# A decayed-attention kernel whose keys and queries come from the host also by dimension, with the decay powers made by doubling

## Chip, cores and metric

The kernel runs on one core of a Trainium2 chip. The metric is the device time of one launch in microseconds, before against after. It does attention and then two mixture-of-experts layers, in one program.

## What is computed

Only the attention part is touched by the change. B = 2 batches, H = 8 heads, S = 768 tokens, D = 48 dimensions, all float32:

```python
state = zeros(B, H, D, D)
for t in range(S):
    cur = einsum('bhd,bhe->bhde', u * k[t], v[t])
    y[t] = einsum('bhd,bhde->bhe', r[t], state + cur)
    state = w[..., None] * state + einsum('bhd,bhe->bhde', k[t], v[t])
```

Its result, as rows of B * S tokens by 384, goes through a layer of 8 experts with one expert to a token, and then through a second one with a capacity.

## The kernel before

The program is written engine by engine, with semaphores set by hand. Each engine's instructions run in the order in which its block writes them.

**Units.** Attention is cut into 12 units of 128 tokens (`NU` = 12); unit n is batch n % 2, chunk n // 2. `units` (L355) writes units 0 to 3 out and loops over the rest, four to a pass. A ring of four buffers holds the loaded r, k and v, 192 KB each, by token (`k_raw`, `r_raw`, `v_raw`; `load`, L403). The heads stand in four pairs g, and in a pair j = 0, 1 lie in partitions 0 to 47 and 64 to 111.

**What a unit does.** With decay w per dimension, a chunk is computed as matrices: k times w to a negative power and r times w to a positive one, so that their product holds the decay between two tokens.

- POOL (GpSimd), L553: `prod1` = r u, `prod2` = `prod1` k, then `r_sc` = r times a table of powers for the next unit (`scale_r`, L546), then `sc`, the diagonal matrices of the bonus of all eight heads, 128x1024 (L568).
- DVE (VectorE), L842: `bonus` = sum of `prod2` over dimensions (L813), `k_sc` for the next unit (L807), `st_sum` (L819) = state plus the update in PSUM, the causal mask, which copies the scores over the lower part of `sc` (L832), and the state's decay (L825).
- PE (TensorE), L1122: turns of `k_sc` and `r_sc` into PSUM (`turn_kr`, L1068 and L1072), the rows of unit n - 2 (L1090), the state update (L1081), the state's part of the values (L1100), the masked scores' part (L1106), the scores of unit n (L1118).
- ACT (ScalarE), L708: copies the turned k and r from PSUM (`kT`, `rT`), the finished rows (`x_rows`, `lg_parts`) and `yT`; in units 1 to 3 it also rounds a third of the first expert's second weight (`w_hi`, `split_high`), for which it waits on the load of that weight.

**Who waits for whom.** `bonus` of unit n waits for `prod2` of n and for the diagonal of n - 1, which read the same tile; the diagonal of n waits for `bonus` of n. The mask of n waits for the scores and the diagonal of n; the values of n for the mask. POOL's `prod1` of n + 1 waits for `bonus` of n.

**Setup.** POOL clears and fills constants; DVE makes the powers with four scans and a reciprocal (L787, L790); PE turns them and ACT copies them to two tables (`k_tab`, `r_tab`). 50 bf16 matmuls ahead of it (`keep_clock`) have no other use than to keep PE busy. Behind attention the routing of layer 1 starts from the last rows.

## Time and profile before

| what | us |
|---|---|
| median of 3 runs | 395.46 (395.17 to 395.58) |
| the profiled execution, whole | 396.4 |
| its span | 394.3 |
| of it PE busy | 366.7 (93%) |
| POOL busy | 184.5 (47%) |
| DVE busy | 209.6 (53%) |
| ACT busy | 133.0 (34%) |

The span is from the first to the last instruction that the profiler saw; the execution's own time is 2.1 us more. An engine's busy share is a mean over stages of different kinds: attention (some 0 to 82 us of the span), the routing, and the two layers. An instruction that waits inside the engine, after its semaphores, counts as busy in its row.

### The profile page before, as it was taken

The page shows a single profiled execution, that of the slowest core. Times are in us where ns is not written, and L with a number is a line of the kernel's source. Part 1 is how long each engine was busy: PE and PEld are TensorE (multiplying, and loading weights), DVE is VectorE, ACT ScalarE, POOL GpSimd, SP SyncE. Part 2 cuts the span into 40 slices and gives each one's busy share as a digit, 9 for nine tenths or more (in the row PEclk, how much of TensorE's full clock was granted, in tenths as well). Part 3 has the DMA queues.
Part 4 walks back from the last instruction along what each step waited for, and adds up shares of the span by engine and source line. Part 5 has one row for each costly group of instructions (what it writes and reads, how often), then busy time and mean ns, then how long its engine had stood idle before and what let it go on. Part 6 is the DMA issues. An engine that isn't in the chain of part 4 may idle for free.

```text
span 394.3 us, 10784 instructions
## 1 busy us (share of the span) xinstructions
PE 366.7 (93%) x3406; PEld 356.9 (91%) x3407; DVE 209.6 (53%) x539; ACT 133.0 (34%) x230; POOL 184.5 (47%) x303
## 2 busy tenths in 40 slices
PE   4689999988999999999999999879999999999990
PEld 4579999977899999999999999769999999999990
DVE  4356666689688655555555577474214454244210
ACT  2447554410544222222222252105215555255220
POOL 6798999815455532323232334152434524444311
PEclk9999999998999999999999999699999999999996
DMA  6898774146999511111111321139349998492000
GB/s 128 142 353 185 164 161 100 40 129 169 402 405 404 215 40 40 40 40 40 40 40 40 112 114 40 13 82 403 122 153 350 317 327 299 136 345 98 27 23 17
DMA packets 68238, 62.08 MB, mean 157 GB/s; under 512 B 45493, under 2 KB 61028, under 8 KB 68080
## 3 DMA queue, kind: packets, MB, share of 16 engines
q1 hardware_dynamic: 63904, 51.26, 40.9%
q0 software_dynamic: 3744, 10.23, 7.9%
q8 instruction: 17, 0.28, 0.3%
q10 hardware_dynamic: 560, 0.21, 0.2%
q14 instruction: 13, 0.11, 0.1%
HBM read 52.85 MB, written 10.14 MB: 160 GB/s over the span
## 4 chain that ended last, share of the span: by engine, by line
PE 82%; DMA 6%; SPq 4%; DVE 3%; issue 2%; ACT 1%; POOL 1%; ACTq 0%; POOLq 0%; DVEq 0%
PE p_h L1203 35%; PE p_o L1225 28%; DMA w_sb<-in_moe_w 3%; PE p_sc L1118 3%; SPq L406 3%; PE p_x L1090 3%; PE p_xt L1180 2%; PE p_y L1100 2%; PE p_y L1106 2%; DMA w_raw<-in_moe_w 2%; PE p_kv L1081 1%; PE p_kt L1068 1%; PE p_rt L1072 1%; PE p_o L1050 1%; DMA xg<-x_rows,src_idx 1%
## 5 line engine op out<-in xcount | busy, mean ns | idle before, releaser
L1203 PE MATMUL p_h<-xT,w_sb 128*128 128x128 f32 x1296 | 149.3, 275 | 1.6 <-ACT xT L670 1.0
L1203 PEld LDWEIGHTS p_h<-xT,w_sb 128*128 128x128 f32 x1296 | 148.2, 192 | 2.3 <-issue 1.3
L982 DVE SCALAR_TENSOR_TENSOR h_lo<-p_h,h_hi 128x512 fp32r<-128x512 f32 x54 | 37.4, 692 | 78.9 <-ACT h_hi L753 77.8
L999 DVE CUSTOM_DVE_ANT_0 lg_prod<-y_row,wg_all 128x384 f32<-128x384 f32 x112 | 55.8, 554 | 41.9 <-ACT y_row L763 41.7
L1225 PE MATMUL p_o<-w_hi,h_hi 128*128 x216 | 75.4, 349 | 0.0
L1225 PE MATMUL p_o<-w_lo,h_hi 128*128 x216 | 73.1, 339 | 0.0
L1225 PE MATMUL p_o<-w_hi,h_lo 128*128 x216 | 73.0, 338 | 0.0
L753 ACT ACTIVATE h_hi<-p_h 128x512 fp32r<-128x512 f32 x54 | 32.3, 598 | 112.2 <-PE p_h L1203 112.2
L580 POOL TENSOR_TENSOR dst_mark<-zeros 128x1 f32<-128x1 f32 x54 | 15.7, 290 | 105.8 <-DVE y_row L999 68.6
L839 DVE TENSOR_TENSOR w_lo<-w_raw,w_hi 128x1024 fp32r<-128x1024 f32 x36 | 42.0, 1221 | 7.8 <-ACT w_hi L670 7.8
L580 POOL TENSOR_TENSOR src_mark<-zeros 128x1 f32<-128x1 f32 x54 | 18.8, 348 | 49.1 <-PE p_xt L1180 33.9
L1225 PEld LDWEIGHTS p_o<-w_hi,h_hi 128*128 128x128 f32 x216 | 40.6, 188 | 0.3 <-issue 0.2
L1225 PEld LDWEIGHTS p_o<-w_lo,h_hi 128*128 128x128 f32 x216 | 40.6, 188 | 0.0
L1225 PEld LDWEIGHTS p_o<-w_hi,h_lo 128*128 128x128 f32 x216 | 40.5, 188 | 0.0
L763 ACT ACTIVATE y_row<-p_o,gate_slot 128x384 f32<-128x384 f32 x27 | 15.7, 582 | 69.0 <-PE p_o L1225 69.0
L670 ACT ACTIVATE w_hi<-w_raw 128x1024 fp32r<-128x1024 f32 x36 | 35.8, 1056 | 4.1 <-DMA w_raw<-in_moe_w 3.8
L595 POOL DMA_INDIRECT xg<-x_rows,src_now x27 | 29.8, 1102 | 6.1 <-issue 4.5
L568 POOL TENSOR_TENSOR sc<-ident,bonus 128x1024 f32<-128x1024 f32 x12 | 25.9, 2162 | 0.8 <-DVE bonus L813 0.8
L832 DVE COPY_PREDICATED sc<-causal,p_sc 128x1024 f32<-128x1024 int32 x12 | 16.0, 1335 | 11.4 <-POOL sc L568 11.4
L670 ACT ACTIVATE xT<-p_xt 128x384 f32<-128x384 f32 x29 | 14.1, 487 | 18.8 <-PE p_xt L1180 18.5
L1050 PE MATMUL p_o<-before_b,ones_b 128*128 128x128 bf16 x254 | 19.2, 244 | 0.9 <-DVE last_tile L949 0.9
L607 POOL DMA_INDIRECT x_rows<-y_row,dst_now x15 | 15.2, 1013 | 8.5 <-issue 8.5
(183 smaller groups left out, 408.9 us busy)
## 6 DMA issues: line engine op xcount, KB each, us to landing
...
k_raw<-in_k SPq DMA_DIRECT2D x12, 192.0 KB, 3.2
r_raw<-in_r SPq DMA_DIRECT2D x12, 192.0 KB, 3.6
v_raw<-in_v SPq DMA_DIRECT2D x12, 192.0 KB, 3.8
x_rows<-x_rows SPq DMA_DIRECT2D x12, 192.0 KB, 1.9
...
```

The source lines that it names most:

```text
L568: gp.tensor_tensor(sc[b][:, :, :, :], ident[:, :].unsqueeze(1).unsqueeze(2).broadcast_to([P, 2, HP, T]), bonus[:, :].rearrange("p (g j) -> ...
L580: gp.tensor_tensor(of[:, :], zeros[:, 0:1], zeros[:, 0:1], ALU.add).then_inc(signal, 1)
L595: gp.indirect_dma_start(out=xg[par][:, 0:width], out_offset=None, in_=src[:, :], in_offset=bass.IndirectOffsetOnAxis(ap=rows, axis=0))\
L670: copy = lambda o, i: sa.activation(o, i, ACT.Copy)
L753: sa.activation(h_hi[:, n * FH:(n + 1) * FH, :], p_h[n][:, :, :], ACT.Relu).then_inc(h_high[layer], 1)
L832: nv.copy_predicated(sc[b][:, :, :, :], low, p_sc[:, :, :, :]).then_inc(masked, 1)
L839: tt(w2_lo[:, at:at + PCW], w2_raw[place][:, n * PCW:(n + 1) * PCW], w2_hi[:, at:at + PCW].bitcast(F32), ALU.subtract).then_inc(w2_ready, 1)
L982: stt(h_lo[:, at, :], p_h[n][:, :, :], 0.0, h_hi[:, at, :].bitcast(F32), ALU.max, ALU.subtract).then_inc(h_ready[layer], 1)
L999: last = nv.tensor_tensor_reduce(out=lg_prod[:, n, :], in0=y_row[par][:, 0:DM], in1=wg2_all[:, e, :], op0=ALU.mult, op1=ALU.add, scale=1.0 ...
L1050: mm(at[:, 0:P], ones_b[:, :], before_b[:, :], start=(n == 0), stop=(n == count - 1))
L1203: last = mm(p_h[half][:, f, :], w1_sb[place][:, c, col:col + P], xT[:, c, :], start=(c == 0), stop=(c == DC - 1))
L1225: last = mm(p_o[:, 0:DM], lhs[:, f, :], rhs[:, here], start=(f == 0 and m == 0), stop=(f == FC - 1 and m == 2))
```

## The change

- The host lays r, k and v side by side by token (`rkv`, one DMA of 128 x 4608 bytes a unit into `nat`), and k and r a second time by dimension (`kr_by_dim`, into `krT`, 112 partitions x 4096 bytes). w comes already one to a partition, in one DMA.
- PE no longer turns k and r. DVE makes `kT` and both halves of `rT` from `krT` and tables of powers, all in SBUF. The state update needs k by token still: `k_sc` moves from DVE to POOL; `r_sc` goes.
- The diagonal is halved: POOL makes j = 0, ACT j = 1 with four activations whose scale is a column of `bonus`. The decay moves from DVE to ACT, four activations a unit, and `st_sum` becomes `acc`, one to a batch.
- `mask` of unit n comes in DVE's unit n + 1, ahead of `kT` and `rT` of n + 1. PE starts a unit with rows(n - 2).
- The powers are made by six doublings (`grow`). ACT copies them into `pr` and `pk`; only `pk` is turned, behind the first scores.
- Clearing is dealt out between DVE and POOL; `zeros`, `ones_e` and the iotas are made by POOL behind attention. `w_hi` of the first expert is made by ACT behind attention.

Where the instructions stand now. DVE, one unit of the loop over units, before (rows between the instructions are register and wait work):

```order
L813 TENSOR_REDUCE bonus<-prod 128x8
L807 TENSOR_TENSOR k_sc<-k_raw,k_tab 128x8x48
L819 TENSOR_TENSOR st_sum<-st,p_kv 128x192
L829 REGISTER_ALU
L831 MEMSET gate_in 128x1
L832 COPY_PREDICATED sc<-causal,p_sc 128x1024
L823 REGISTER_ALU
L825 TENSOR_TENSOR st<-st_sum,pw 128x4x48
```

and now:

```order
L822 TENSOR_REDUCE bonus<-prod 128x8
L835 MEMSET gate_in 128x1
L836 COPY_PREDICATED sc<-causal,p_sc 128x1024
L807 TENSOR_TENSOR kT<-krT,pk 112x512
L814 TENSOR_TENSOR rT<-krT,pr 48x512 x2
L828 TENSOR_TENSOR acc<-st,p_kv 128x192
```

`k_sc` and the decay are gone, and `kT` and two `rT` stand between the mask and the state's sum. POOL, one unit of the loop, before:

```order
L555 TENSOR_TENSOR prod<-r_raw,u_tab 128x384
L556 ISA
L557 TENSOR_TENSOR prod<-prod,k_raw 128x384
L548 ISA
L550 TENSOR_TENSOR r_sc<-r_raw,r_tab 128x8x48
L566 REGISTER_ALU
L53 REGISTER_ALU
L568 TENSOR_TENSOR sc<-ident,bonus 128x1024
```

and now:

```order
L537 TENSOR_TENSOR prod<-nat,u_tab 128x384
L538 ISA
L539 TENSOR_TENSOR prod<-prod,nat 128x384
L543 REGISTER_ALU
L53 REGISTER_ALU
L545 TENSOR_TENSOR sc<-ident,bonus 128x512
L552 TENSOR_TENSOR k_sc<-nat,k_tab 128x8x48
```

`r_sc` is gone, `k_sc` stands last, and the diagonal has 512 columns in place of 1024. PE, from its first matmuls to the scores of the first unit before:

```order
L1050 MATMUL p_x<-before_b,ones_b 128x128 x50
L1057 MATMUL p_kt<-ident,pk 128x112 x4
L1057 MATMUL p_rt<-ident,pr 128x112 x4
L1068 MATMUL p_kt<-ident,k_sc 112x128 x4
L1072 MATMUL p_rt<-ident,r_sc 112x128 x4
L1050 MATMUL p_x<-before_b,ones_b 128x128 x12
L1118 MATMUL p_sc<-rT,kT 128x128 x8
```

and now to the scores of the second:

```order
L1071 MATMUL p_warm<-before_b,ones_b 128x128 x50
L1131 MATMUL p_sc<-rT,kT 128x128 x8
L1081 MATMUL p_tab<-ident,pk 128x112 x4
L1071 MATMUL p_warm<-before_b,ones_b 128x128 x12
L1109 MATMUL p_y<-rT,st 64x128 x8
L1119 MATMUL p_y<-sc,nat 64x128 x8
L1091 MATMUL p_kv<-nat,k_sc 64x48 x8
L1131 MATMUL p_sc<-rT,kT 128x128 x8
```

The scores of unit 0 (the first L1131) now stand ahead of the only turn of powers (L1081).

The diff, cut to its core:

```diff
-                for to, src in ((k_raw[q][:, :, :], k_t), (r_raw[q][:, :, :], r_t), (heads(v_raw[q]), v_t)):
-                    sp.dma_start(to, src[b, bass.ds(c, 1), :, :, :].rearrange("n t h d -> (n t) h d"))\
-                        .then_inc(raw_loaded[q], 16)
+                sp.dma_start(nat[q][:, 0:3 * W], rkv_t[b, bass.ds(c, 1), :, :].rearrange("n t x -> (n t) x"))\
+                    .then_inc(nat_loaded[q], 16)
+                sp.dma_start(krT[q][0:R, :, :, :], kr_t[b, bass.ds(c, 1), :, :, :, :].rearrange("n p x g t -> (n p) x g t"))\
+                    .then_inc(krT_loaded[q], 16)
...
-                    sp.wait_ge(r_scaled, n + 1)
+                    sp.wait_ge(kT_ready, n + 1)
+                    sp.wait_ge(rT_ready, n + 1)
...
+            def products(i, q, n):
+                pool.wait_ge(nat_loaded[q], 16 * (i + 1))
+                wait_pos(pool, bonus_sum, n)
+                gp.tensor_tensor(prod1[:, :, :], r_nat(q), u_tab[:, :, :], ALU.mult).then_inc(bonus_prod, 1)
+                pool.wait_ge(bonus_prod, 2 * n + 1)
+                gp.tensor_tensor(prod2[:, :, :], prod1[:, :, :], k_nat(q), ALU.mult).then_inc(bonus_prod, 1)
+            def diagonal(n, b):
+                pool.wait_ge(bonus_sum, n + 1)
+                wait_pos(pool, y_made, n - 1)
+                gp.tensor_tensor(sc[b][:, 0, :, :], ident[:, :].unsqueeze(1).broadcast_to([P, HP, T]),
+                                 bonus[:, :].rearrange("p (g j) -> p j g", j=2)[:, 0, :].unsqueeze(2).broadcast_to([P, HP, T]),
+                                 ALU.mult).then_inc(diag_pool, 1)
+            def scale_k(q, n, b):
+                wait_pos(pool, kv_made, n - 1)
+                gp.tensor_tensor(k_sc[b][:, :, :, 0:D], k_nat(q).rearrange("p (g j) d -> p g j d", j=2),
+                                 k_tab[:, :, :, 0:D], ALU.mult).then_inc(k_scaled, 1)
+            def unit(i, q, n, b, c):
+                products(i, q, n)
+                if isinstance(n, int) and n == 0:
+                    pool.wait_ge(cleared, 2)
+                    pool.wait_ge(k_tab_ready, 1)
+                    scale_k(q, n, b)
+                else:
+                    diagonal(n, b)
+                    scale_k(q, n, b)
+            pool.wait_ge(u_loaded, 16)
+            units(pool, unit)
...
-                wait_pos(pool, bonus_sum, n)
-                gp.tensor_tensor(prod1[:, :, :], r_raw[q][:, :, :], u_tab[:, :, :], ALU.mult).then_inc(bonus_prod, 1)
-                pool.wait_ge(bonus_prod, 2 * n + 1)
-                gp.tensor_tensor(prod2[:, :, :], prod1[:, :, :], k_raw[q][:, :, :], ALU.mult).then_inc(bonus_prod, 1)
-                if q < RING - 1:
...
-                pool.wait_ge(bonus_sum, n + 1)
-                wait_pos(pool, y_made, n - 1)
-                gp.tensor_tensor(sc[b][:, :, :, :], ident[:, :].unsqueeze(1).unsqueeze(2).broadcast_to([P, 2, HP, T]),
-                                 bonus[:, :].rearrange("p (g j) -> p j g", j=2).unsqueeze(3).broadcast_to([P, 2, HP, T]),
-                                 ALU.mult).then_inc(bonus_diag, 1)
...
+            act.dma_start(u_tab[:, :, :], u.partition_broadcast(P)).then_inc(u_loaded, 16)
...
+            act.wait_ge(grown, 7)
+            copy(pr[:, :, M + 1:T], grow[:, 0, :, 0:M - 1])
+            copy(pr[:, :, 0:M], grow[:, 1, :, M - 1::-1]).then_inc(powers_ready, 1)
+            copy(pk[:, :, M:T], grow[:, 1, :, :])
+            copy(pk[:, :, 0:M - 1], grow[:, 0, :, M - 2::-1]).then_inc(powers_ready, 1)
+            act.wait_ge(powers_turned, 1)
+            copy(k_tab[:, :, :, :].rearrange("p g j d -> p g (j d)")[:, :, 0:R], p_tab[:, :, 0:R]).then_inc(k_tab_ready, 1)
...
+            def decay(n, b):
+                act.wait_ge(summed, n + 1)
+                act.wait_ge(y_made, n + 1)
+                for g in range(HP):
+                    last = sa.activation(st[b][:, g, 0:D], acc[b][:, g, :], ACT.Copy, scale=w_T[:, g:g + 1])
+                last.then_inc(decayed, 1)
+            def diagonal(n, b):
+                act.wait_ge(bonus_sum, n + 1)
+                wait_pos(act, y_made, n - 1)
+                for g in range(HP):
+                    last = sa.activation(sc[b][:, 1, g, :], ident[:, :], ACT.Copy, scale=bonus[:, 2 * g + 1:2 * g + 2])
+                last.then_inc(diag_act, 1)
...
-                copy(kT[0:R, :, :], p_kt[0:R, :, :]).then_inc(kT_ready, 1)
-                wait_pos(act, y_made, n - 1)
-                for j in range(2):
-                    at = slice(HD * j, HD * j + D)
-                    last = copy(rT[b][at, j, :, :], p_rt[at, :, :])
...
+                diagonal(n, b)
                 if not (isinstance(n, int) and n < 2):
                     rows(n - 2, b, c - 1)
                 if not (isinstance(n, int) and n < 1):
                     y_out(n - 1)
-                if isinstance(n, int) and 0 < n <= NPC:
-                    split_high(0, 0, [n - 1])
+                    decay(n - 1, 1 - b)
...
+            split_high(0, 0)
...
-            def scale_k(i, q, n, b):
-                dve.wait_ge(raw_loaded[q], 48 * (i + 1))
-                wait_pos(dve, kv_made, n - 1)
-                tt(k_sc[b][:, :, :, 0:D], pairs(k_raw[q]), k_tab[:, :, :, 0:D], ALU.mult).then_inc(k_scaled, 1)
...
+            dve.wait_ge(w_loaded, 16)
+            nv.tensor_copy(grow[:, 0, :, 0:1], w_col[:, :].unsqueeze(2))
+            nv.reciprocal(grow[:, 1, :, 0:1], w_col[:, :].unsqueeze(2)).then_inc(grown, 1)
+            for n in range(6):
+                m = 1 << n
+                dve.wait_ge(grown, n + 1)
+                tt(grow[:, :, :, m:2 * m], grow[:, :, :, 0:m], grow[:, :, :, m - 1:m].broadcast_to([P, 2, HP, m]),
+                   ALU.mult).then_inc(grown, 1)
+            dve.wait_ge(grown, 7)
+            dve.wait_ge(cleared, 2)
+            def scale_kT(i, q, n, b):
+                dve.wait_ge(krT_loaded[q], 16 * (i + 1))
+                wait_pos(dve, scored, n - 1)
+                tt(kT[b][0:R, :, :], krT[q][0:R, 0, :, :], pk[0:R, :, :], ALU.mult).then_inc(kT_ready, 1)
+            def scale_rT(q, n, b):
+                wait_pos(dve, y_made, n - 1)
+                for j in range(2):
+                    at = slice(HD * j, HD * j + D)
+                    last = tt(rT[b][at, j, :, :], krT[q][at, 1, :, :], pr[at, :, :], ALU.mult)
+                last.then_inc(rT_ready, 1)
...
-                wait_pos(dve, bonus_diag, n)
+                wait_pos(dve, diag_pool, n)
+                wait_pos(dve, diag_act, n)
...
-            def state_decay(n, b):
-                dve.wait_ge(state_ready, 2 * n + 1)
-                dve.wait_ge(y_made, n + 1)
-                tt(st[b][:, :, 0:D], st_sum[:, :, :], decay, ALU.mult).then_inc(state_ready, 1)
+                wait_pos(dve, decayed, n - 1)
+                tt(acc[b][:, :, :], st[b][:, :, 0:D], p_kv, ALU.add).then_inc(summed, 1)
...
+                dve.wait_ge(diag_act, n + 1)
...
             def unit(i, q, n, b, c):
-                bonus_of(n)
-                if q < RING - 1:
-                    scale_k(i, q + 1, n + 1, 1 - b)
+                if isinstance(n, int) and n == 0:
+                    dve.wait_ge(krT_loaded[0], 16)
+                    tt(kT[0][0:R, :, M:T], krT[0][0:R, 0, :, M:T], grow[0:R, 1, :, :], ALU.mult)
+                    tt(kT[0][0:R, :, 0:M - 1], krT[0][0:R, 0, :, 0:M - 1], grow[0:R, 0, :, M - 2::-1], ALU.mult)
+                    nv.tensor_copy(kT[0][0:R, :, M - 1:M], krT[0][0:R, 0, :, M - 1:M]).then_inc(kT_ready, 1)
+                    dve.wait_ge(powers_ready, 1)
+                    scale_rT(q, n, b)
+                    bonus_of(n)
+                    tt(w_T[:, :], grow[:, 0, :, M - 1], grow[:, 0, :, M - 1], ALU.mult)
+                    dve.wait_ge(bonus_sum, 1)
+                    dve.wait_ge(consts, 2)
+                    tt(sc[0][:, 0, :, :], ident[:, :].unsqueeze(1).broadcast_to([P, HP, T]),
+                       bonus[:, :].rearrange("p (g j) -> p j g", j=2)[:, 0, :].unsqueeze(2).broadcast_to([P, HP, T]),
+                       ALU.mult).then_inc(diag_pool, 1)
+                elif isinstance(n, int) and n == 1:
+                    dve.wait_ge(powers_ready, 2)
+                    scale_kT(i, q, n, b)
+                    mask(n - 1, 1 - b)
+                    scale_rT(q, n, b)
+                    state_sum(n - 1, 1 - b)
+                    bonus_of(n)
                 else:
-                    if isinstance(i, int):
-                        scale_k(i + 1, 0, n + 1, 1 - b)
-                    else:
-                        with dve.If(i < NU // RING - 1):
-                            scale_k(i + 1, 0, n + 1, 1 - b)
-                if not (isinstance(n, int) and n < 1):
+                    bonus_of(n)
+                    mask(n - 1, 1 - b)
+                    scale_kT(i, q, n, b)
+                    scale_rT(q, n, b)
                     state_sum(n - 1, 1 - b)
-                mask(n, b)
-                if not (isinstance(n, int) and n < 1):
-                    state_decay(n - 1, 1 - b)
-            scale_k(0, 0, 0, 0)
             units(dve, unit)
-
+            mask(NU - 1, (NU - 1) % B)
+            dve.wait_ge(consts, 3)
...
-                    last = turn(p_t[:, g, 0:R], t[0:R, g, :], ident[0:R, 0:R])
+                    last = turn(p_tab[:, g, 0:R], pk[0:R, g, :], ident[0:R, 0:R])
...
-                pe.wait_ge(raw_loaded[q], 48 * (i + 1))
+                wait_pos(pe, summed, n)
+                pe.wait_ge(nat_loaded[q], 16 * (i + 1))
...
-            def values(q, n, b):
-                pe.wait_ge(rT_ready, n + 1)
-                wait_pos(pe, state_ready, 2 * n - 2)
+            def inter(n, b):
+                wait_pos(pe, decayed, n - 1)
...
+            def values(i, q, n, b):
+                pe.wait_ge(nat_loaded[q], 16 * (i + 1))
                 pe.wait_ge(masked, n + 1)
...
-                        last = mm(p_sc[:, j, g, :], kT[at, g, :], rT[b][at, j, g, :], start=True, stop=True)
+                        last = mm(p_sc[:, j, g, :], kT[b][at, g, :], rT[b][at, j, g, :], start=True, stop=True)
...
-                turn_kr(n, b)
                 if isinstance(n, int) and n == 0:
-                    keep_clock(p_x[:, 0, :], WARM_TURN)
-                if not (isinstance(n, int) and n < 2):
+                    score(n, b)
+                    turn_powers()
+                    keep_clock(p_warm[:, 0, :], WARM_TURN)
+                elif isinstance(n, int) and n == 1:
+                    inter(n - 1, 1 - b)
+                    values(0, 0, n - 1, 1 - b)
+                    state(0, 0, n - 1, 1 - b)
+                    score(n, b)
+                else:
+                    before = i if q else i - 1
+                    if isinstance(n, int) and n == 2:
+                        pe.wait_ge(small_in, 16 * N_SMALL)
+                        pe.wait_ge(cleared, 2)
                     rows(n - 2)
-                if not (isinstance(n, int) and n < 1):
-                    state(i if q else i - 1, (q - 1) % RING, n - 1, 1 - b)
-                    values((q - 1) % RING, n - 1, 1 - b)
-                score(n, b)
+                    state(before, (q - 1) % RING, n - 1, 1 - b)
+                    inter(n - 1, 1 - b)
+                    values(before, (q - 1) % RING, n - 1, 1 - b)
+                    score(n, b)
...
+    laid = {"rkv": np.stack([r, k, v]).transpose(1, 3, 0, 2, 4)}
+    rows = np.arange(HD) % D
+    kr = np.stack([k, r]).reshape(2, B, H // 2, 2, S // T, T, D).transpose(1, 4, 3, 6, 0, 2, 5)
+    laid["kr_by_dim"] = kr[:, :, :, rows].reshape(B, S // T, 2 * HD, 2, H // 2, T)[:, :, 0:HD + D]
+    laid["w_by_dim"] = w.reshape(H // 2, 2, D).transpose(1, 2, 0)[:, rows].reshape(2 * HD, H // 2)
```

## Rows read from the trace of the kernel before

**Rows 1.** Busy time by stretch: start:end us, length, PE, PEld, DVE, ACT, POOL, PEclk, DMA.

```profile
10.00:20.00 10.00, 6.85 (x88) 5.71 (x90) 3.58 (x7) 4.31 (x8) 8.01 (x7) 1.00 0.82 141
...
50.00:60.00 10.00, 10.00 (x156) 9.33 (x152) 6.74 (x12) 5.22 (x12) 9.84 (x9) 1.00 0.68 144
```

**Rows 2.** Chain that ended last: start us, length us, engine, tile and line.

```profile
16.86 8.38 DMA w_raw<-in_moe_w
...
26.22 0.59 ACT kT L670
...
27.98 1.16 PE p_sc L1118 x16
...
60.21 1.09 PE p_sc L1118 x16
61.30 0.58 PE p_kt L1068 x4
61.88 0.44 PE p_rt L1072 x4
62.32 0.89 PE p_x L1090 x8
...
65.57 1.09 PE p_sc L1118 x16
...
76.29 1.09 PE p_sc L1118 x16
```

**Rows 3.** Timeline, POOL and DVE in one unit: start, length, engine, line, operation.

```profile
60.00 2.22 POOL L568 TENSOR_TENSOR sc<-ident,bonus 128x1024 f32<-128x1024 f32 x1
...
62.17 1.00 POOL L555 TENSOR_TENSOR prod<-r_raw,u_tab 128x384 f32<-128x384 f32 x1
...
63.25 1.01 POOL L557 TENSOR_TENSOR prod<-prod,k_raw 128x384 f32<-128x384 f32 x1
63.56 0.91 DVE L825 TENSOR_TENSOR st<-st_sum,pw 128x192 f32<-128x192 f32 x1
...
64.22 1.12 POOL L550 TENSOR_TENSOR r_sc<-r_raw,r_tab 128x384 f32<-128x384 f32 x1
...
64.86 0.89 DVE L807 TENSOR_TENSOR k_sc<-k_raw,k_tab 128x384 f32<-128x384 f32 x1
65.30 2.21 POOL L568 TENSOR_TENSOR sc<-ident,bonus 128x1024 f32<-128x1024 f32 x1
```

**Rows 4.** Timeline, the same instructions where the other engine is quiet.

```profile
11.62 0.56 DVE L807 TENSOR_TENSOR k_sc<-k_raw,k_tab 128x384 f32<-128x384 f32 x1 [1.30 <-ACT r_tab L670]
...
15.03 0.99 POOL L550 TENSOR_TENSOR r_sc<-r_raw,r_tab 128x384 f32<-128x384 f32 x1
...
15.10 0.55 DVE L813 TENSOR_REDUCE bonus<-prod 128x8 f32<-128x384 f32 x1 [2.92 <-POOL prod L557]
...
75.61 1.90 POOL L568 TENSOR_TENSOR sc<-ident,bonus 128x1024 f32<-128x1024 f32 x1 [0.76 <-DVE bonus L813]
...
78.86 0.33 DVE L825 TENSOR_TENSOR st<-st_sum,pw 128x192 f32<-128x192 f32 x1
```

**Rows 5.** Instructions by line on DVE: operation, shapes, count, busy us, mean ns.

```profile
L839 DVE TENSOR_TENSOR w_lo<-w_raw,w_hi 128x1024 fp32r<-128x1024 f32 x36 | 42.0, 1221 | 7.8 <-ACT w_hi L670 7.8
...
L832 DVE COPY_PREDICATED sc<-causal,p_sc 128x1024 f32<-128x1024 int32 x12 | 16.0, 1335 | 11.4 <-POOL sc L568 11.4
...
L819 DVE TENSOR_TENSOR st_sum<-st,p_kv 128x192 f32<-128x192 f32 x11 | 3.8, 342 | 0.0
...
L780 DVE MEMSET k_sc<- 128x512 f32 x2 | 1.0, 485 | 1.0 <-PEq L1272 0.9
```

**Rows 6.** Issues of DMAs: KB each, us to landing.

```profile
k_raw<-in_k SPq DMA_DIRECT2D x12, 192.0 KB, 3.2
```

**Rows 7.** Timeline, end of attention and ScalarE's next wait.

```profile
82.64 0.19 ACT L670 ACTIVATE lg_parts<-p_x 128x32 f32<-128x32 f32 x1
...
86.07 0.21 ACT L670 ACTIVATE plan_ends<-ends 1x8 int32<-1x8 f32 x1 [3.25 <-DVE ends L905]
```

More of the change, by code:

```diff
@@ L164, in chain_program @@
             gate_in = sa("gate_in", [P, 1])
-            st_sum = sa("st_sum", [P, HP, D])
+            acc = [sa(f"acc{b}", [P, HP, D]) for b in range(B)]
             st = [sa(f"st{b}", [P, HP, HD]) for b in range(B)]
@@ L280, in chain_program @@
         cleared = sem("cleared")
-        raw_loaded = [sem(f"raw_loaded{q}") for q in range(RING)]
-        r_scaled = sem("r_scaled")
+        krT_loaded = [sem(f"krT_loaded{q}") for q in range(RING)]
+        nat_loaded = [sem(f"nat_loaded{q}") for q in range(RING)]
         k_scaled = sem("k_scaled")
@@ L348, in chain_program @@
         wg2_spread = sem("wg2_spread")
[L350 to L351 removed]
+        N_SMALL, N_ROUTER = 2, 4
+        W = H * D
+        part = lambda q, x: nat[q][:, x * W:(x + 1) * W].rearrange("p (h d) -> p h d", d=D)
+        r_nat, k_nat, v_nat = (lambda q: part(q, 0)), (lambda q: part(q, 1)), (lambda q: part(q, 2))
         rows_of = lambda j: slice(HD * j, HD * j + HD)
[L353 removed]
         def units(eng, unit):
@@ L572, in _ @@
-            pool.wait_ge(tables_ready, 2)
-            scale_r(0, 0, 0, 0)
-            units(pool, unit)
+            pool.wait_ge(consts, 3)
+            pool.wait_ge(zeros_set, 1)
             def mark(of, signal):
@@ L778, in _ @@
             over_c = lambda a, n: a.unsqueeze(1).broadcast_to([P, n, a.shape[1]])
-            for t in k_sc:
-                last = nv.memset(t[:, :, :, :], 0.0)
-            last.then_inc(cleared, 1)
-            dve.wait_ge(consts, 1)
-            dve.wait_ge(w_loaded, 32)
-            nv.memset(pw[:, :, 0:1], 1.0)
-            for g in range(HP):
-                last = nv.tensor_tensor_scan(pw[:, g, 1:T + 1], w_col[:, g:g + 1].broadcast_to([P, T]),
-                                             zeros[:, 0:T], 1.0, ALU.mult, ALU.add)
@@ new lines, in _ @@
+            nv.memset(eye_wg1[:, :, :], 0.0).then_inc(ones_set, 1)
+            nv.memset(k_sc[0][:, :, :, :], 0.0)
+            for t in st:
+                nv.memset(t[:, :, :], 0.0)
+            for q in range(RING):
+                nv.memset(nat[q][:, 3 * W:], 0.0)
+            nv.memset(pr[:, :, M:M + 1], 1.0)
+            nv.memset(pk[:, :, M - 1:M], 1.0).then_inc(cleared, 1)
+            dve.wait_ge(w_loaded, 16)
+            nv.tensor_copy(grow[:, 0, :, 0:1], w_col[:, :].unsqueeze(2))
```

158 lines of the change are left out of this document (50 added, 108 removed).

## The prediction

> **What bounds the kernel now.** I read the chain that ended last first. From 28 to 77 us it never leaves PE: scores at 60.21, turns of k (0.58) and of r (0.44), rows (0.89), and so on to the next scores at 65.57, a lap of 5.36 us [rows 2]. Before 28 us it goes through the load of `w_raw`, for which ACT waited ahead of a `kT` that PE needed [rows 2]. The stretches confirm it: between 50 and 60 us PE is busy 10.00 of 10 us [rows 1]. But POOL is at 9.84 of 10 there [rows 1], so the second view is the timeline of POOL and DVE. The reader is to see two things. POOL's own lap, diagonal to diagonal, is 65.30 - 60.00 = 5.30 us, hardly under PE's. And the two engines lengthen each other. The state's decay (DVE, 128x192) takes 0.91 us when `prod2` is running and 0.33 when POOL is quiet; `k_sc` 0.89 against 0.56; the diagonal 2.22 against 1.90 [rows 3, 4]. The decay was issued at 63.56 and ended at 64.47, so its 0.33 us began at 64.14, when `prod2`, begun at 63.25, had worked 0.89 us. The decay's 192 columns hold POOL off for 0.20, to 64.34. `k_sc` ended at 65.75, so it began at 65.19, when `r_sc` had worked 0.85. These operations run one after the other. A 384-column product of POOL holds DVE off for 0.85 to 0.89 us, I take 0.88; DVE's `k_sc` holds POOL off for its 384 columns, 0.40. `bonus` (one input) and the mask and the state's sum (one input in PSUM) don't show it: their rows have the same length all through [rows 4, 5].
>
> The Trainium skill has two rules for this. "Advanced Engine Details and Errata", VectorE Performance Modes, names only GpSimd and DVE's 2-port forms as blocking each other; a float32 product of two tensors is none of them, and by that rule alone the new operations would run free. "SBUF — State Buffer", Who interferes with whom, adds DVE instructions with two SBUF inputs against GpSimd instructions that read SBUF. Rows 3 speak for the second; what the first would give is a rival below.
>
> **PE.** Both turns go: 5.36 - 0.58 - 0.44 = 4.34 us a unit [rows 2]. If PE stayed the bound, 12 x 1.02 = 12.2 us would be won. It doesn't stay.
>
> **POOL and DVE, one lap.** DVE gets three products with both inputs in SBUF, 512 columns each, in place of `k_sc` (384) and the decay (192). From 384 columns in 0.56 and 1024 in 1.22 us [rows 4, 5] a column costs 1.03 ns: 0.69 us as a row, 0.53 of it holding POOL off. POOL keeps two products, takes `k_sc` for `r_sc`, and halves the diagonal: 1.90 / 2, less 0.02 of overlap, 0.93 us (bounds: 0.88, as fast as its products; 1.0, if the fixed part is large). I go from one `bonus` to the next:
>
> - `bonus` seen by POOL 0.07, diagonal 0.93, `k_sc` 0.88. Beside these two DVE makes the mask (1.34 [rows 5]), so it comes to `kT` while `k_sc` runs and waits for it.
> - `kT` 0.53, `prod1` 0.88, first `rT` 0.53, `prod2` 0.88, second `rT` 0.53 and 0.06 to the next instruction. I take them alternately, since each engine's next request waits while the other works.
> - the state's sum 0.34 less 0.06 of overlap, 0.28, then `bonus` 0.54 [rows 4, 5].
>
> Sum 6.11 us. The same arithmetic on the lap before (`prod1` to `prod2` 1.08, `prod2` 0.89, decay 0.20, `r_sc` 0.85, `k_sc` 0.40, diagonal 1.87) gives 5.29, where the trace has 5.30. Before, `bonus` lay beside `r_sc`; now POOL has nothing to do while DVE sums, since the next diagonal needs `bonus` and `k_sc` is behind it. PE's scores need the second `rT` and last 1.16, ending 0.4 us after `bonus`: they set the mask, not the lap. If DVE kept all three products together, the lap would be 5.9 to 6.0; if each handover cost 0.08 more, 6.4.
>
> **Start.** DVE clears some 2600 columns at 0.485 / 512 us [rows 5], 2.5 us, and is done at about 4.2 with the small ones. The first loads land 3.2 us after issue or somewhat later [rows 6], so r and k by token are in at about 5.0. The doublings are 504 columns in six dependent steps, some 1.7 us, and wait behind POOL's first two products, 0.8 each: 7.8. `kT` of unit 0 to 8.6, `rT` to 9.9, scores to 11.2. Only then does PE turn `pk` (0.6, as the turns [rows 2]), ACT copies it (0.5), and POOL, which has waited for `k_tab` with everything behind it, makes `k_sc` at 12.3. Two products and an `rT` between them to 15.9, the second `rT`, sum and `bonus` of unit 1 to 17.3; then diagonal, `k_sc` and two products free of DVE to 21.3; `bonus` of unit 2 to 21.9. From there the full lap: the scores of unit 2 begin at 27.3. Before they began at 27.98 [rows 2]: the earlier start and ACT's wait on `w_raw`, which goes, are used up by the longer way from unit 0 to 2. Bounds: 25.5 to 29.5, for loads and clearing.
>
> **End.** Eight laps: scores of unit 10 at 27.3 + 48.9 = 76.2. Unit 11 has no products beside it: scores 1.16 and 0.05, mask 1.26, three products 0.60, 0.60, 0.69, handover 0.1, together 4.5. Its scores begin at 80.7, against 76.29 before [rows 2]: **4.4 us later**. Values and rows behind them are as before.
>
> **What costs nothing.** ACT loses `kT` and `rT` and gets eight small activations a unit. Between 0.19 (32 columns) and 0.59 (512) [rows 7, 2] they cost 1.5 to 4.7 us; by the slope, some 2.2, so ACT is busy 3.6 of 6.1 us. Were it 4.7, ACT would come to the lap itself. The three `w_hi` behind attention: twice 0.59 is an upper bound, 3.6 us in all, by the slope 3.05; ACT is idle from 82.83 to 86.07, 3.24 us [rows 7]: nothing, or 0.3. Loads grow from 590 KB to 1.05 MB a unit; at 144 GB/s with the DMA engines busy 0.68 [rows 1], full use would give 212 GB/s, 5.0 us a unit, under the lap and four units ahead, and rows of 4 KB should do better than pieces of 192 bytes. SP's load for unit n + 4 now also waits for `kT` and `rT`, which come before the values it waits for anyway. Clock: granted 1.00 between 10 and 20 us with PE busy 6.85 of 10 [rows 1]; PE will be busy 4.34 of 6.11, 7.1 of 10, so I leave it at the upper level, 2.4 GHz. Routing and experts shift as they are.
>
> **Sum.** The profiled execution took 396.4 us (span 394.3), 0.9 over the median of 395.46. Plus 4.4 it would take 400.8; from the median, **399.9 us**. Its own range, from laps of 5.9 to 6.4 (8 x -0.2 to 8 x +0.3) and the start's -1.8 to +2.2: 396.5 to 404.
>
> **Rivals.**
>
> - *The products don't block each other in their new forms.* For it: the new ones are whole rows of 512 and `rT` lies in 48 partitions; none of these forms is in the trace. Against: `k_sc` and the decay, two inputs in SBUF as well, are blocked in each unit. POOL's lap would be 0.93 + 0.93 + 1.08 + 0.99 + 0.05 + 0.54 + 0.07 = 4.6, with PE at 4.34 inside it, and the start some 3.8 us shorter: 23.5 + 8 x 4.6 + 4.6 = 64.9 against 76.29, that is 384. It decides as soon as less than 0.5 of the 1.6 us of DVE's products stands in POOL's way. That is also what the skill's narrower rule would give. Chance 0.14.
> - *A short lap and a short start.* The least lap with blocking is POOL's 3.6, DVE's 1.6 and `bonus` 0.54 without any wait: 5.75; then 8 x -0.36 = -2.9, and with a start 1 to 3 us better (loads of long rows, faster clearing) the time is 394 to 396. It needs everything to mesh. Chance 0.16, half of it faster.
> - *The clock falls.* PE now has one gap of some 1.8 us in each lap. At 1.2 GHz its 4.34 become 8.7 us, 12 x (8.7 - 6.1) = 31 us on top: 430. Against it: the same share without a fall [rows 1]. Chance 0.02.
> - *The changed path is no path:* that would be PE still at 5.36; the turns are gone from its program, so I give it nothing.
>
> **Chances.** Forecast 0.68, the others 0.14, 0.16, 0.02. A measurement of this kernel tells about 0.2% from no change, 0.8 us. Faster by over 0.2%: 0.14 + 0.08 = 0.22. Within: 0.08. Slower: 0.70. The range reaches down over the short lap and start to 393 and leaves out the first and third rival, 0.16: 393 to 404.
>
> **What would show it.** Right: `kT` and `rT` on DVE with rows of 0.8 to 1.6 us in place of 0.69; `prod1` and `prod2` at 1.4 in place of 1.0; about 6.1 us from one scores to the next; POOL idle once a lap for `bonus`; PE idle some 1.8 us ahead of the scores; the first `k_sc` near 12 us; the last scores near 81. Wrong: rows of 0.69 and 1.0 beside each other, or a lap under 5.4.

## The result, and the profile after

The changed kernel took **408.1 us** (median of 4 runs, 407.03 to 409.3) against 395.52 for the kernel before on the same chip: a ratio of 1.031, 95% interval 1.028 to 1.034. It is 3.1% slower. The profiled execution took 408.8 us with a span of 407.1 us, against 396.4 and 394.3 before. Forecast were 399.9 us and a range of 393 to 404, so the sign was right and the size was not: the change cost 12.6 us where I had 4.4.

The busy time by stretch, whose columns are those of [rows 1]; the last four columns are POOL, the granted clock, the DMA share and GB/s:

```profile
10.00:20.00 10.00, 6.02 (x52) 5.38 (x54) 5.92 (x12) 1.71 (x5) 3.97 (x5) 0.66 1.04 250
...
30.00:40.00 10.00, 7.84 (x76) 7.06 (x72) 8.36 (x11) 3.35 (x11) 6.11 (x6) 0.54 0.90 332
40.00:50.00 10.00, 8.70 (x142) 7.85 (x138) 8.11 (x11) 6.44 (x22) 7.42 (x7) 1.00 0.76 232
50.00:60.00 10.00, 6.62 (x103) 5.84 (x99) 8.98 (x13) 4.84 (x17) 6.90 (x7) 0.99 0.63 197
60.00:70.00 10.00, 10.00 (x114) 9.22 (x116) 8.09 (x10) 4.87 (x18) 7.77 (x8) 0.67 0.45 151
```

Two things are new against [rows 1]. Between 50 and 60 us PE is busy 6.62 of 10 us, where it was busy all the time, and DVE has become the fullest engine. And the clock, 1.00 in both stretches of [rows 1], is 0.66, 0.54 and 0.67 in three of these.

The chain that ended last, which answers to [rows 2]: start, length, what.

```profile
1.76 9.09 DMA krT<-in_kr_by_dim
...
13.43 2.08 PE p_sc L1131 x16
15.51 0.95 PE p_tab L1081 x4
...
32.53 2.08 PE p_sc L1131 x16
...
52.38 1.16 PE p_sc L1131 x16
53.54 1.08 PE p_x L1100 x8
54.62 0.60 PE p_kv L1091 x16
55.23 0.89 PE p_y L1109 x16
56.11 0.88 PE p_y L1119 x16
56.99 1.69 issue
58.68 1.16 PE p_sc L1131 x16
59.84 2.00 PE p_x L1100 x8
...
89.53 1.16 PE p_sc L1131 x16
```

The lap from one scores to the next is 58.68 - 52.38 = 6.30 us, of which PE works 4.61 and waits 1.69. The same `p_x` takes 1.08 us at the upper level of the clock (2.4 GHz) and 2.00 at the lower one (1.2 GHz). The last scores start at 89.53 us, 13.2 later than in [rows 2]. The span grew by 12.8, so the loss lies in attention; 0.4 us of it came back behind.

The timeline of one lap, POOL and DVE, which answers to [rows 3]:

```profile
53.20 1.04 POOL L545 TENSOR_TENSOR sc<-ident,bonus 128x512 f32<-128x512 f32 x1 [1.47 <-DVE bonus L822]
...
53.59 1.31 DVE L836 COPY_PREDICATED sc<-causal,p_sc 128x1024 f32<-128x1024 int32 x1 [0.46 <-issue]
...
54.20 1.00 POOL L552 TENSOR_TENSOR k_sc<-nat,k_tab 128x384 f32<-128x384 f32 x1
...
54.81 0.95 DVE L807 TENSOR_TENSOR kT<-krT,pk 112x512 f32<-112x512 f32 x1
...
55.17 1.45 POOL L537 TENSOR_TENSOR prod<-nat,u_tab 128x384 f32<-128x384 f32 x1
...
55.68 2.89 DVE L814 TENSOR_TENSOR rT<-krT,pr 48x512 f32<-48x512 f32 x2
...
56.70 1.32 POOL L539 TENSOR_TENSOR prod<-prod,nat 128x384 f32<-128x384 f32 x1
...
58.60 0.35 DVE L828 TENSOR_TENSOR acc<-st,p_kv 128x192 f32<-128x192 f32 x1
...
58.88 0.54 DVE L822 TENSOR_REDUCE bonus<-prod 128x8 f32<-128x384 f32 x1
...
59.50 1.04 POOL L545 TENSOR_TENSOR sc<-ident,bonus 128x512 f32<-128x512 f32 x1 [1.48 <-DVE bonus L822]
```

The picture of the forecast is there: `rT` x2 takes 2.89 us, where two free ones take 1.38 (below), `prod1` and `prod2` 1.45 and 1.32 in place of 1.0, and POOL is idle 1.48 us a lap for `bonus`. As a sum, with the forecast in brackets: `bonus` seen 0.08 (0.07), diagonal 1.00 (0.93), `k_sc` 0.89 (0.88), then alternately `kT`, `prod1`, `rT`, `prod2` and `rT` 3.35 (3.35), handover to `acc` 0.16 (0.06), `acc` 0.28 (0.28), `bonus` 0.54 (0.54): 6.30 (6.11). From the start of `k_sc` to the sum the rows give 4.40 us (4.29); how these divide into `k_sc`, turns and handover is worked out with the forecast's lengths of a turn.

The start, POOL's and DVE's timelines:

```profile
4.84 1.66 DVE L798 TENSOR_TENSOR grow<-grow 128x8 f32<-128x8 f32 x6
...
9.23 0.99 POOL L537 TENSOR_TENSOR prod<-nat,u_tab 128x384 f32<-128x384 f32 x1 [4.75 <-DMA nat<-in_rkv]
...
10.97 0.60 DVE L852 TENSOR_TENSOR kT<-krT,grow 112x256 f32<-112x256 f32 x1 [4.47 <-DMA krT<-in_kr_by_dim]
...
11.90 1.38 DVE L814 TENSOR_TENSOR rT<-krT,pr 48x512 f32<-48x512 f32 x2
...
17.17 1.00 POOL L552 TENSOR_TENSOR k_sc<-nat,k_tab 128x384 f32<-128x384 f32 x1 [5.87 <-ACT k_tab L665]
```

The powers are done at 6.5 us. DVE then waits 4.47 us and POOL 4.75 us for the first loads. `k_sc` of unit 0 begins at 17.2 us, where the forecast had 12.3.

### The profile page after: what moved, and what is told of

Same layout as the page of the kernel before. It is cut to its first block, busy times and chain, and to the rows that moved or that the text cites. A ratio compares the mean times of both kernels' runs of the same rounds, so it can differ in the third digit from the quotient of the medians.

```text
span 407.1 us, 10604 instructions
## 1 busy us (share of the span) xinstructions
PE 368.2 (90%) x3306; PEld 357.9 (88%) x3307; DVE 231.8 (57%) x563; ACT 137.2 (34%) x287; POOL 175.2 (43%) x294
## 4 chain that ended last, share of the span: by engine, by line
PE 81%; DMA 6%; issue 4%; DVE 4%; POOL 1%; ACT 1%; SPq 0%; ACTq 0%; DVEq 0%; POOLq 0%
PE p_h L1226 34%; PE p_o L1248 27%; PE p_sc L1131 4%; PE p_x L1100 3%; DMA w_sb<-in_moe_w 3%; PE p_y L1119 3%; PE p_y L1109 3%; PE p_xt L1203 2%; DMA krT<-in_kr_by_dim 2%; PE p_o L1071 2%; PE p_kv L1091 2%; DMA xg<-x_rows,src_idx 1%; DVE rT L814 1%; PE p_sl L1170 1%; DVE sc L836 0%
## 5 line engine op out<-in xcount | busy, mean ns | idle before, releaser
L590 POOL DMA_INDIRECT xg<-x_rows,src_now x27 | 28.9, 1070 | 6.1 <-issue 4.3
L1131 PE MATMUL p_sc<-rT,kT 48*128 48x128 f32 x192 | 15.9, 310 | 15.4 <-issue 10.1
L1131 PEld LDWEIGHTS p_sc<-rT,kT 48*128 48x128 f32 x192 | 13.7, 212 | 18.1 <-issue 18.1
L814 DVE TENSOR_TENSOR rT<-krT,pr 48x512 f32<-48x512 f32 x24 | 28.4, 1183 | 0.2
```

The source lines that it names most:

```text
L590: gp.indirect_dma_start(out=xg[par][:, 0:width], out_offset=None, in_=src[:, :], in_offset=bass.IndirectOffsetOnAxis(ap=rows, axis=0))\
L814: last = tt(rT[b][at, j, :, :], krT[q][at, 1, :, :], pr[at, :, :], ALU.mult)
L1131: last = mm(p_sc[:, j, g, :], kT[b][at, g, :], rT[b][at, j, g, :], start=True, stop=True)
```

## The experiments

Theory 1 was from the start that the products of DVE and POOL exclude each other (the lap); the open questions were what the two misses, the late start and the low clock, cost. A lap runs from the scores of one unit to those of the next, and below it is taken from the weight loads of the scores, which start some hundredths of a microsecond ahead of the rows shown.

### The factor of DVE's products in PSUM

```diff
+            p_pk = pb("p_pk", [P, HP, T])
+            p_pr = pb("p_pr", [P, HP, T])
...
-            copy(pr[:, :, 0:M], grow[:, 1, :, M - 1::-1]).then_inc(powers_ready, 1)
+            copy(p_pr[:, :, 0:M], grow[:, 1, :, M - 1::-1]).then_inc(powers_ready, 1)
...
-    krT[q][0:R, 0, :, :], pk[0:R, :, :], ALU.mult)
+    krT[q][0:R, 0, :, :], p_pk[0:R, :, :], ALU.mult)
```

and the same for `rT` with `p_pr`.

> The changed kernel with its two power tables in PSUM, so that each of DVE's three products of a unit has one input in SBUF. Theory 1 (DVE's products with two SBUF inputs and POOL's operations run one after the other, and this makes the lap of 6.3 us): kT and rT rows fall from 0.95 to 1.5 to about 0.75 us, POOL's products from 1.45 and 1.32 to 1.0, the lap from scores to scores from 6.30 to 4.6 to 4.9; over ten laps some 15 us, so 390 to 395 us. Theory 2 (the lap is the chain through bonus, whatever the port): rows and lap within 0.3 us of what they are, 405 to 409 us.

Measured: 392.79 us, ratio to before 0.9915 (0.9875 to 0.9954), 15.3 us less than the changed kernel. Its timeline, the same instructions:

```profile
53.32 1.37 DVE L817 TENSOR_TENSOR rT<-krT,p_pr 48x512 f32<-48x512 f32 x2
...
53.64 1.01 POOL L537 TENSOR_TENSOR prod<-nat,u_tab 128x384 f32<-128x384 f32 x1
...
54.73 1.00 POOL L539 TENSOR_TENSOR prod<-prod,nat 128x384 f32<-128x384 f32 x1
...
57.46 0.66 DVE L810 TENSOR_TENSOR kT<-krT,p_pk 112x512 f32<-112x512 f32 x1
57.48 1.01 POOL L552 TENSOR_TENSOR k_sc<-nat,k_tab 128x384 f32<-128x384 f32 x1
```

and its stretch:

```profile
50.00:60.00 10.00, 9.70 (x152) 8.84 (x154) 8.32 (x15) 7.01 (x24) 8.43 (x9) 1.00 1.03 272
```

`kT` (0.66) and `k_sc` (1.01) run beside each other at full length, and so do `rT` and the products. The lap is 4.73 us (two earlier ones take 5.44 and 5.29), and PE is busy 9.70 of 10 us between 50 and 60. Work, sizes and order of a unit are those of the changed kernel, only where one factor lies differs (in setup ScalarE makes two copies more), so the exclusion is the cause of the long lap: this is shown. With the long lap the low clock behind it went too, 1.00 in each stretch from 20 to 80 us, so the 15.3 us are the worth of both. By the Trainium skill, "SBUF — State Buffer", Who interferes with whom, a DVE instruction outside the 2-port modes with at most one SBUF input doesn't contend with GpSimd, and one with two contends with a GpSimd instruction that reads SBUF; both halves are in these two traces. The narrower rule that the prediction took from the Trainium skill, "Advanced Engine Details and Errata", VectorE Performance Modes, and by which these forms would run free (its first rival), doesn't hold for them.

### The diagonal wholly on POOL

In units 1 to 11 POOL makes both halves (1024 columns) and ScalarE none:

```diff
-                gp.tensor_tensor(sc[b][:, 0, :, :], ...
+                gp.tensor_tensor(sc[b][:, :, :, :], ...
...
-                diagonal(n, b)
+                if isinstance(n, int) and n == 0:
+                    diagonal(n, b)
```

> The changed kernel with the diagonal wholly on POOL again from unit 1 on (1024 columns), nothing of it on ACT. Theory 1 (POOL's operations, DVE's products and bonus stand one behind the other in the lap): the diagonal takes 1.9 us, the lap grows by 0.85, from 6.30 to 7.15, the last scores come 7 to 9 us later, 415 to 418 us. Theory 2 (the lap is DVE and PE alone): lap within 0.3 us of 6.30, the time within 2 us of 408.

Measured, in a single run: 414.75 us. The lap is 6.78 us, not 7.15. Its timeline says why:

```profile
61.97 1.90 POOL L545 TENSOR_TENSOR sc<-ident,bonus 128x1024 f32<-128x1024 f32 x1 [0.67 <-DVE bonus L824]
...
63.03 1.39 DVE L808 TENSOR_TENSOR kT<-krT,pk 112x512 f32<-112x512 f32 x1
...
63.83 1.45 POOL L552 TENSOR_TENSOR k_sc<-nat,k_tab 128x384 f32<-128x384 f32 x1
...
66.76 1.33 POOL L539 TENSOR_TENSOR prod<-prod,nat 128x384 f32<-128x384 f32 x1
...
67.26 0.35 DVE L830 TENSOR_TENSOR acc<-st,p_kv 128x192 f32<-128x192 f32 x1
```

With the longer diagonal `kT` comes first and `k_sc` waits for it; the alternation is shifted by one, the second `rT` comes ahead of `prod2`, and the sum runs under `prod2`. The serial sum is then 0.08 + 1.90 + 0.53 + 0.88 + 0.53 + 0.88 + 0.53 + 0.88 + 0.55 = 6.76. So the method of the forecast holds to 0.02 us, but only with the order of turns read from this trace. Moving half of the diagonal to ScalarE gains 0.48 us a lap here.

### The half diagonal and w_hi alone, in the kernel before

Two kernels. In the first ScalarE's `w_hi` goes behind attention, in the second ScalarE also makes half the diagonal:

```diff
-                if isinstance(n, int) and 0 < n <= NPC:
-                    split_high(0, 0, [n - 1])
...
             rows(NU - 1, (NU - 1) % B, (NU - 1) // B)
+            split_high(0, 0)
```

```diff
+                act.wait_ge(bonus_sum, n + 1)
+                for g in range(HP):
+                    last = sa.activation(sc[b][:, 1, g, :], ident[:, :], ACT.Copy, scale=bonus[:, 2 * g + 1:2 * g + 2])
+                last.then_inc(diag_act, 1)
```

> The kernel before with one part of the change alone: w_hi of the first expert made by ACT behind attention. Theory 1 (ACT's wait for w_raw held PE up once, from about 26 to 28 us, and ACT is idle 3.2 us behind attention): 1.5 to 2 us faster, 393.5 to 394. Theory 2 (the gap is made up later, or the three activations delay the routing): 395 to 396.5.

> The kernel before, with the rounding of the first expert's weight behind attention (as before_whi) and only the second half of the diagonal moved to ScalarE, as the change has it. Nothing else of the change. Theory 1 (PE's 5.36 us a unit sets the lap of the kernel before, POOL's row only looks full since it waits inside): POOL's busy time between 50 and 60 us falls from 9.84 to some 8 of 10 us, the lap stays 5.36, the last scores start near 76.3 and the time is that of before_whi, 394.5 us within 0.8. Theory 2 (POOL and PE set it together, 5.30 and 5.36, and hold each other up): the lap falls under 5.36, by up to 0.1 us, and the time to 393.5. Rival: ScalarE's four activations of the diagonal come ahead of the copies of the turned k and r that PE waits for: lap 5.5 to 5.8, time 396 to 399 us.

Measured: 394.5 us (ratio 0.996, 0.993 to 0.999) and 394.28 (0.9964, 0.9937 to 0.9992). `w_hi` behind attention gains about 0.4%, near the resolution and between the two ranges expected; its trace doesn't show where, for its last scores start at 76.33 us, against 76.29 before. The half diagonal on top gains nothing more. The stretch of the second:

```profile
50.00:60.00 10.00, 10.00 (x156) 9.24 (x154) 6.96 (x11) 8.02 (x20) 8.25 (x9) 1.00 0.69 149
```

POOL's busy time falls from 9.84 [rows 1] to 8.25 and the steady lap stays 5.36 us: PE alone set it, and POOL's full row was a follower. So of the change's parts only the removal of the turns shortens what bounded the steady lap, and it pays only if the new products of DVE don't wait for POOL's.

### The clock: idle matmuls in the gaps

130 instead of 50 idle matmuls in setup, and 16 ahead of each scores from unit 2 on:

```diff
-WARM_PLAN, WARM_FIRST = 50, 12
+WARM_PLAN, WARM_FIRST = 130, 12
...
+                    keep_clock(p_tab[:, 0, :], 16)
                     score(n, b)
```

> The changed kernel with 130 in place of 50 bf16 matmuls in the setup and 16 of them in PE's gap ahead of each scores. Theory 1 (the fall of PE's clock to half in four stretches costs 1.3 us in a lap, about 5 to 8 us in all): granted clock 1.00 to 95 us, all full laps 6.3 us, the last scores 5 to 8 us earlier, 400 to 403 us. Theory 2 (PE has slack in the lap, the clock costs nothing at the end): the last scores move less than 1.5 us, 406.5 to 409 us.

Measured: 406.64 us, 1.0249 (1.0196 to 1.0302), and the last scores at 87.88, 1.6 us earlier than in the changed kernel. The 5 to 8 us of theory 1 did not come. The clock is 1.00 between 50 and 60 us with PE busy 8.61 of 10, but 0.70 between 20 and 30. With the clock held in setup the scores of unit 2 start at 30.7 us, 1.8 earlier, and the lap behind them takes 5.57 us in place of 7.67. The next two take 7.47 and 6.89, and from there they are 6.3 as before. A new wait came up, POOL's timeline:

```profile
36.39 1.00 POOL L537 TENSOR_TENSOR prod<-nat,u_tab 128x384 f32<-128x384 f32 x1 [2.78 <-DMA nat<-in_rkv]
```

The load of unit 4 was issued at 23.78 us, behind the first expert's weights, and took 12.45. In the changed kernel, where the scores of unit 2 are later, POOL doesn't wait for it.

### The loads: unit 0 first, and the expert's weights last

In one kernel SP waits for the loads of unit 0 before it issues unit 1's, and for those before the rest. In another the first expert's weight loads stand behind the ring's reloads. A third joins the latter with the idle matmuls.

```diff
                 load(q, q % B, q // B)
+                if q < 2:
+                    sp.wait_ge(nat_loaded[q], 16)
+                    sp.wait_ge(krT_loaded[q], 16)
```

```diff
-            expert_w2(0, 0, 0)
-            expert_w1(0, 0, 0)
...
                     store(n, b, c)
+            expert_w2(0, 0, 0)
+            expert_w1(0, 0, 0)
```

> The changed kernel with SP waiting for the loads of unit 0 before it issues those of unit 1, and for those of unit 1 before the rest. Theory 1 (eight loads in flight share the DMA engines, so the first lands late): the first krT lands at 6 to 7.5 us in place of 10.85, the first scores begin 3 to 4 us earlier, 403.5 to 406 us. Theory 2 (one load takes that long by itself, its rate or its latency): it lands at 9 or later and later units suffer, 408 to 411 us.

> The changed kernel with the first expert's two weight loads issued behind the ring's reloads instead of ahead of them. In the run with the filled clock the first product of unit 4 waited 2.8 us for its load, which stood behind these 3 MB. Theory 1 (in the changed kernel itself the fall of the clock between 26 and 39 us hides that wait, so the clock is what costs there): the last scores move less than 1 us, 407 to 409 us. Theory 2 (the load is what holds it up): the last scores come 2 to 3 us earlier, 404.5 to 406.5 us.

> Both together: weight loads behind the reloads, 130 matmuls in the setup and 16 in each gap. Theory (clock and load each cover the other, so that only both edits together give the time back): granted clock 1.00 but for one stretch near 25 us, no wait for a load from unit 2 on, full laps of 6.3 us from the scores of unit 2 at 30.8: the last scores at 30.8 + 8 x 6.3 + 4.7 = 86, 404 to 405.5 us, 3 to 4 under the changed kernel. Rival (each does its part alone): no more than the filled clock alone, 406.6.

Measured: 409.94 us (1.0332, 1.0278 to 1.0385), 408.41 (1.0306, 1.0251 to 1.036) and 405.82 (1.023, 1.0176 to 1.0284). The first one's chain:

```profile
1.75 7.36 DMA krT<-in_kr_by_dim
```

With unit 0's two loads (1.05 MB) alone of the ring in flight, `krT` still lands only at 9.1 us, as theory 2 had it, not at 5. The other loads in flight cost 1.7 us of the lateness. The rest is there with these two alone; how much of it is their size is not shown, since the DMA engines were busy only 0.41 and 0.11 of the last two microseconds ahead of the landing. What was won at the first scores (12.3) was lost later, since all other loads came later. Late weights alone change nothing (408.41 against 408.1): the granted clock was 0.50 between 10 and 20 us and 0.51 between 30 and 40. With the idle matmuls as well it is 2.6 us less than with late weights alone, taken beside it on the same chip, and 2.3 less than the changed kernel, of 3.5 expected. The rival, no more than the idle matmuls alone give (406.64), is not excluded: the intervals of the two ratios overlap, and the last scores start at 88.4 us, not earlier than the 87.9 there. The lap from unit 2 to unit 3 was 8.75 us, with the clock at 0.66 between 30 and 40 us.

### All together, with the factor in PSUM

PSUM factor, late weights and 130 idle matmuls in setup; then the same with idle matmuls inside units 1 to 3; then in unit 2 alone (20 ahead of the rows, 20 ahead of the masked part, 8 ahead of the scores).

```diff
+                    if lead:
+                        keep_clock(p_tab[:, 0, :], 20)
                     rows(n - 2)
...
+                    if lead:
+                        keep_clock(p_tab[:, 0, :], 20)
                     values(before, (q - 1) % RING, n - 1, 1 - b)
+                    if lead:
+                        keep_clock(p_tab[:, 0, :], 8)
                     score(n, b)
```

> The tables in PSUM, with the weight loads behind the reloads and 130 matmuls in the setup. Port theory: laps of 4.73 us throughout from the scores of unit 2, where the kernel with the tables alone had 5.44 and 5.29 behind late loads; with unit 2 at 27.5 to 29 the last scores are at 70 to 71.7, 388 to 390.5 us. Rival (with a lap this short the loads of 1 MB a unit are the bound wherever the weights stand): laps over 5 us stay, 391 to 393 us.

> The changed kernel with power tables in PSUM, late weight loads and 130 warm matmuls in setup (as psum_late, 390.6 us), and in units 1 to 3 short runs of the same idle bf16 matmuls in PE's gaps (12 before the scores of unit 1; 20 before the rows, 20 before the masked part and 10 before the scores of units 2 and 3). Question: in psum_late the lap from the scores of unit 2 to those of unit 3 took 7.74 us, with the granted clock at 0.50 from 28 to 34 us. Theory 1 (the low clock alone makes that lap long): the clock stays at 1.00 between 20 and 40 us, the lap is 4.7 to 5.2, the last scores start at 70 to 71 in place of 72.7 and the time is 388.0 to 389.0 us. Theory 2 (the load of unit 3 or 4 holds it, the clock only shows it): the clock stays up, the lap stays over 7 and the time is 390.6. Rival: the idle matmuls stand in the way of the chain yT, rows, mask, values, since PE runs in order: laps 1 to 3 grow by 0.5 to 1 us each and the gain is halved or gone, 389.5 to 391.

> As psum_hold, but with idle matmuls only in unit 2 (20 before the rows, 20 before the masked part, 8 before the scores), where PE had gaps of 1.70, 1.51 and 0.72 us in psum_late, and none in units 1 and 3. In psum_hold the clock stayed at 1.00, yet the lap from the scores of unit 2 to those of unit 3 was 7.68 us: PE ran through without a gap, 3.0 us of it idle matmuls. Theory 1 (what made that lap long was the clock in psum_late and the idle matmuls in psum_hold; nothing else holds it): clock 1.00 from 20 to 40 us, unit 1 to 2 some 8.0 us, unit 2 to 3 4.7 to 5.0, last scores near 69.3, time 387 to 388 us. Theory 2 (the activity of unit 3 alone lets the clock fall again): granted clock under 0.8 between 30 and 40 us, lap over 5.5, time 389 to 390.5. Theory 3 (a load or a buffer holds unit 3): clock 1.00, lap over 6 with PE idle in it, time 390.

Measured: 390.6 us (0.9849, 0.9804 to 0.9893), 392.14 (0.9909, 0.9881 to 0.9937) and 389.94 (0.9847, 0.9814 to 0.988). All three beat both kernels. The first missed its 388 to 390.5 us narrowly, the second lies above all that was expected of it. PE's gaps in unit 2 of the first, and its stretches between 20 and 40 us:

```profile
22.21 1.12 PE L1103 MATMUL p_x<-eye_wg,yT 112*128 112x120 f32 x8 [1.70 <-ACT yT L665]
...
26.34 1.09 PE L1122 MATMUL p_y<-sc,nat 128*64 128x128 f32 x16 [1.51 <-DVE sc L839]
28.16 2.06 PE L1134 MATMUL p_sc<-rT,kT 48*128 48x128 f32 x16 [0.72 <-issue]
```

```profile
20.00:30.00 10.00, 6.06 (x82) 5.29 (x78) 4.81 (x9) 6.28 (x21) 8.15 (x9) 0.91 0.54 172
30.00:40.00 10.00, 10.00 (x127) 9.23 (x126) 6.95 (x12) 4.68 (x17) 7.61 (x8) 0.75 0.51 176
```

of the second:

```profile
30.00:40.00 10.00, 10.00 (x165) 9.10 (x164) 6.61 (x11) 4.97 (x17) 7.89 (x8) 1.00 0.56 194
```

and of the third:

```profile
20.00:30.00 10.00, 9.06 (x138) 7.90 (x138) 5.06 (x10) 5.89 (x20) 7.94 (x8) 1.00 0.59 158
30.00:40.00 10.00, 9.77 (x150) 8.88 (x151) 8.45 (x17) 6.69 (x24) 8.05 (x9) 1.00 0.80 255
```

The lap from unit 2 to 3 is 7.74 us in the first (low clock), 7.68 in the second (clock 1.00, but 3 us of idle matmuls in a PE without a gap) and 4.73 in the third. So the clock fell for the gaps in unit 2, where PE waits for ScalarE's `yT` and for DVE's mask, and the next unit pays at 1.2 GHz. The idle matmuls help only in those gaps. Behind its slow lap the first kernel catches up in part: PE runs without a gap, at 4.54 us a lap, for five laps. In the third the last scores start at 71.46 us, 1.3 earlier than in the first, and the span is 388.7 against 390.2. The medians come from two chips and their ratios don't differ. Expected were 387 to 388 us with the last scores near 69.3; the lap from unit 1 to unit 2 took 8.80 us, where 8.0 was expected.

## Why the prediction was wrong

**The bound and its price: right.** PE's steady lap was the bound before, as the kernel with half a diagonal shows; PE waits now, and DVE and POOL set the lap by taking turns. The PSUM kernel shows that the exclusion alone makes 6.30 out of 4.73. For laps without exclusion the first rival had 4.6. PE's own lap without the turns was put too low, at 4.34: where PE runs without a gap it takes 4.54, since the rows behind the scores take 1.08 us and behind the turns took 0.89. Here that costs nothing, as PE waits.

**The lap: two terms too small.** 6.11 forecast, 6.30 measured. The diagonal of 512 columns costs 1.00 on the path, not 0.93 (I had halved 1.90; the bound "1.0, if the fixed part is large" is what came), and from the start of `k_sc` to the sum it is 4.40, not 4.29, which the sum above books as a handover of 0.16 in place of 0.06. Eight laps: 1.5 us.

**The start: "The first loads land 3.2 us after issue or somewhat later [...] so r and k by token are in at about 5.0" failed.** They were in at 9.2, and krT at 10.9. The 3.2 us belong to loads of 192 KB [rows 6]; the new ones have 576 and 448 KB, and eight of them share the DMA engines. The prediction holds a better number itself: "full use would give 212 GB/s, 5.0 us a unit", which I used for the laps and not for the start. It would have been too low still: with unit 0's two loads alone `krT` took 7.36 us. The doublings, which I had put behind POOL's products, were done at 6.5 and off the path.

**The clock: "so I leave it at the upper level, 2.4 GHz" failed.** The argument was one stretch of [rows 1] with PE busy 6.85 of 10 at a clock of 1.00. In the changed kernel 6.62 of 10 is granted 0.99 as well, but the next ten microseconds only 0.67. A busy share alone does not tell; the clock must be read in the stretches that follow. Nor do the gaps alone: in the kernel with late weights the laps are 6.3 us with the same waits of 1.7, and the clock stays at 1.00 from 60 to 90 us, with PE busy 8.31, 6.51 and 8.13 of 10. What decides it these runs don't show. My rival on the clock had all laps at 1.2 GHz, 430 us, with a chance of 0.02. What came lies between: it falls in stretches, and PE at half speed fills its own gap, and there the clock came back.

**How the miss of 8.8 us at the last scores divides** (89.5 against 80.7). The first scores are 3.4 late, 3.2 of it for the loads. They and the turns of the powers run at 1.2 GHz, 0.9 + 0.35 more. With 0.5 from the units between, the scores of unit 2 are 5.2 late (32.5 against 27.3). The eight laps then take 52.2 us in place of 48.9: 1.5 by the lap itself, 1.8 by two laps at the low clock (7.67 and 7.58, each partly made up by a lap of 5.88 behind it). The last lap adds 0.3. The time's miss is 8.2 us. The split between load and clock is worked out from one trace. The runs bear out a part of the clock's share: the clock held in setup brought the scores of unit 2 forward by 1.8 us, but of all that the clock cost no run gave back more than 2.6 us, with low clock left in one stretch. Of the loads' 3.2 us one run took away 1.7, and 1.1 at the first scores; that the loads can be had earlier than that no run shows.

**What costs nothing: right in the steady lap, but for the loads.** ScalarE with eight small activations (half the diagonal 1.26, decay 1.01), and `w_hi` behind attention, are off the chain there; in unit 0 the chain goes through its half of the diagonal, which stands behind `k_tab` (1.27 us from 16.93). The loads of later units were not free: `cap_i`, a load of 1 KB, stands behind the ring's eight loads and blocks SP for 12.98 us, and with it the weights and the reload of unit 4. In the changed kernel no wait comes of it, and late weights alone gain nothing; with the clock held it is a wait of 2.78 us.
